# Batch 0's attention by blocks of 128 features in a fused attention and gated MLP kernel

## What is computed

```python
def _attn_ref(q, k, v):                       # [8, 8, 576, 64] each
    q_s = np.exp(q - np.max(q, axis=-1, keepdims=True))
    q_s = q_s / (np.sum(q_s, axis=-1, keepdims=True) + 1e-09)     # softmax over a head's 64 features
    k_s = np.exp(k - np.max(k, axis=2, keepdims=True))
    k_s = k_s / (np.sum(k_s, axis=2, keepdims=True) + 1e-09)      # softmax over the 576 tokens
    kv = np.einsum('bhsd,bhse->bhde', k_s, v)
    return np.einsum('bhsd,bhde->bhse', q_s, kv)
```

## Time and profile before

| | us |
|---|---|
| median of 3 runs | 949.03 (947.65 to 949.77) |
| the profiled execution | 948.56 |
| its span, first to last instruction | 946.8 |
| PE busy in the span | 923.9 (98%) |
| DVE, ACT, POOL busy | 601.5, 374.9, 361.9 |

### The profile page before, as it was taken

One profiled execution on the slowest core, in us unless ns is written; L12 is line 12 of the kernel. 1 busy time (PEld: TensorE's weight loads), 2 busy tenths in 40 slices (PEclk: granted clock), 3 DMA queues, 4 the chain that ended last, 5 costly groups with the idle time before them and its releaser, 6 DMA issues.

```text
span 946.8 us, 14688 instructions
## 1 busy us (share of the span) xinstructions
PE 923.9 (98%) x5980; PEld 864.1 (91%) x5980; DVE 601.5 (64%) x943; ACT 374.9 (40%) x564; POOL 361.9 (38%) x230
## 2 busy tenths in 40 slices
PE   6899899999999999999999998999999999999998
PEld 5799799899999998999999997999998989999987
DVE  6667666657746666576355797866667666667660
ACT  3561433524524335245234254533434333434331
POOL 4985545446426444464204133322222222232320
PEclk8899999999999999999999999999999999999999
DMA  8815425134061151330412302020202020200001
GB/s 256 251 48 178 134 51 193 37 100 158 12 200 56 45 194 41 99 109 12 134 64 82 111 13 73 12 84 23 73 23 73 23 73 23 84 23 22 25 23 55
DMA packets 50482, 77.84 MB, mean 82 GB/s; under 512 B 4336, under 2 KB 22768, under 8 KB 49520
## 3 DMA queue, kind: packets, MB, share of 16 engines
q1 hardware_dynamic: 45808, 67.48, 22.6%
q10 hardware_dynamic: 4608, 9.44, 2.7%
HBM read 56.97 MB, written 18.89 MB: 80 GB/s over the span
## 4 chain that ended last, share of the span: by engine, by line
PE 89%; DVE 6%; DMA 2%; issue 1%; ACT 1%; POOL 1%; SPq 0%; ACTq 0%; DVEq 0%; POOLq 0%
PE psum L452 51%; PE psum L444 29%; PE psum L510 3%; PE psum L593 2%; PE psum L486 2%; PE psum L545 1%; DMA plain_arena<-in_q 1%; DVE plain_arena L1322 1%; DVE split_arena L1304 1%; DMA x_dram<-plain_arena 1%; DVE plain_arena L1133 0%; DVE plain_arena L1246 0%; DVE split_arena L1462 0%; DVE plain_arena L1320 0%; DVE plain_arena L1215 0%
## 5 line engine op out<-in xcount | busy, mean ns | idle before, releaser
L452 PE MATMUL psum<-split_arena 128*128 128x288 f32 x4032 | 559.0, 297 | 6.0 <-DVE split_arena L1201 2.9
L452 PEld LDWEIGHTS psum<-split_arena 128*128 128x128 f32 x4032 | 545.9, 189 | 12.6 <-DVE split_arena L1201 3.2
L444 PE MATMUL psum<-split_arena 128*128 128x512 f32 x1248 | 298.3, 393 | 2.7 <-DVE split_arena L1462 2.6
L444 PEld LDWEIGHTS psum<-split_arena 128*128 128x128 f32 x1248 | 232.2, 189 | 49.8 <-DVE split_arena L1462 3.5
L1614 POOL TENSOR_TENSOR plain_arena<-plain_arena 128x576 f32<-128x576 f32 x64 | 107.4, 1678 | 281.6 <-ACT plain_arena L915 281.6
L1325 DVE SCALAR_TENSOR_TENSOR plain_arena<-plain_arena 128x576 f32<-128x576 f32 x64 | 96.2, 1503 | 2.2
L1320 DVE TENSOR_SCALAR plain_arena<-plain_arena 128x576 f32<-128x576 f32 x64 | 36.0, 563 | 90.1 <-ACT plain_arena L909 90.1
L1555 POOL TENSOR_TENSOR plain_arena<-plain_arena 128x576 f32<-128x576 f32 x32 | 46.5, 1453 | 110.6 <-DVE plain_arena L1259 110.6
L909 ACT ACTIVATE plain_arena<-psum 128x576 f32<-128x576 f32 x64 | 41.6, 650 | 105.4 <-PE psum L452 74.4
L915 ACT ACTIVATE plain_arena<-plain_arena 128x576 f32<-128x576 f32 x64 | 43.7, 683 | 43.5 <-DVE split_arena L1462 40.4
L1462 DVE TENSOR_TENSOR split_arena<-plain_arena,split_arena 128x576 fp32r<-128x576 f32 x64 | 53.2, 832 | 10.9 <-ACT split_arena L921 10.0
(11 more groups left out here) (80 smaller groups left out, 787.0 us busy)
## 6 DMA issues: line engine op xcount, KB each, us to landing
x_dram<-plain_arena ACTq DMA_DIRECT2D x32, 288.0 KB, 2.1
plain_arena<-x_dram SPq DMA_DIRECT2D x8, 1152.0 KB, 5.7
out_rows<-plain_arena SPq DMA_DIRECT2D x36, 256.0 KB, 2.0
plain_arena<-in_v SPq DMA_DIRECT2D x32, 256.0 KB, 3.3
plain_arena<-in_kT SPq DMA_DIRECT2D x7, 1152.0 KB, 8.0
plain_arena<-in_q SPq DMA_DIRECT2D x7, 1024.0 KB, 5.7
plain_arena<-in_k SPq DMA_DIRECT2D x7, 1024.0 KB, 5.6
plain_arena<-in_w_in SPq DMA_DIRECT2D x8, 512.0 KB, 5.8
```

What stands on the lines that cost most here:

```text
L444: mm = e.matmul(out, stat[s], mov[m], start=first and n == 0, stop=last and n == 2, skip_group_check=True)
L452: mm = e.matmul(out[:, h, 0:NH], stat[s], mov[m][:, h * NH:(h + 1) * NH], start=first and n == 0, stop=last and n == 2, skip_group_check=True)
```

## The change

Only batch 0's attention and what is loaded for it are rewritten. Four things are different.

1. Loading. SP issues, for each block d, kT (128 features x 576 tokens), q and v of the block's 128 columns from two new inputs laid out by block (`q_first`, `v_first`, 128 x 5 x 128, the tail's missing rows filled with repeated ones), and the right half of `w_in`'s rows. The left halves follow. `w_in` is split into its two halves for `hi_w` and `lo_w` too.
2. k. DVE takes the maximum along the free axis of kT, ACT exponentiates with the negated maximum as bias, PE turns the exponentiated block once, and ACT (four tiles) and DVE (the tail) copy it out of PSUM.
3. Per block, the value product (5 matmuls into one bank), the inverse of the sums, the halves of kv (with the scale applied in the same instructions), q's chain and its turning, the piece of x, and with it `v_part(0, 0, [d])` follow each other. `v_part(0, 1)` comes at the end in one piece, since all pieces of x use its banks.
4. Batch 1. `load_kT(1)` moves behind `load_q(1)` and `W_SG[1]`, because kT of batch 0 now lies in its place; the load of `W_SG[0]` no longer waits.

Loading, cut:

```diff
-            for u in range(NU):
-                j, n, rows = UNITS[u][0], len(UNITS[u]), rows_of(u)
-                e.dma_start(kn[0:rows, j:j + n, :],
...
-            for j in range(NJ):
-                load_v(0, j)
             for d in range(DT):
-                load_w(W_IN[d], w_in_raw[d])
+                e.dma_start(k_view[:, d, :], kT[0, d * P:(d + 1) * P, :]).then_inc(kT_first_in[d], 16)
+                e.dma_start(qs_first[:, d, :, :], q_first[d].rearrange("p (j c) -> p j c", j=NJ)).then_inc(q_first_in[d], 16)
+                e.dma_start(vs_first[:, :, d, 0:P], v_first[d].rearrange("p (j c) -> p j c", j=NJ)).then_inc(v_first_in[d], 16)
+                load_w(W_IN[0][d], w_in_raw[0][d])
+            for d in range(DT):
+                load_w(W_IN[1][d], w_in_raw[1][d])
             load_w(W_SG[2], w_sg_raw[2])
-            e.wait_ge(kv_step, NJ - 1)
             load_w(W_SG[0], w_sg_raw[0])
-            load_kT(1)
             load_q(1)
             e.wait_ge(w_lo, 2)
             load_w(W_SG[1], w_sg_raw[1])
+            load_kT(1)
             load_k(1)
```

```diff
+            def turn_first_k(d):
+                e.wait_ge(k0_exp, d + 1)
+                if d > 0:
+                    e.wait_ge(k0_main, d)
+                for j in range(NJ - 1):
+                    mm = e.transpose(ek_turned[:, j * P:(j + 1) * P], k_view[:, d, j * P:(j + 1) * P], ident)
+                mm.then_inc(k0_turned, 1)
+            def turn_first_q(d):
+                e.wait_ge(q0_norm, d + 1)
+                if d > 0:
+                    e.wait_ge(q0_lo, d)
...
+            def kv_first_block(d):
...
+                for j in range(NJ):
+                    mm = e.matmul(kv_first, kn[:, j, d * P:(d + 1) * P], vs_first[:, j, d, :],
+                                  start=j == 0, stop=j == NJ - 1, skip_group_check=True)
+            def x_first(d):
+                e.wait_ge(kv0_lo, 2 * d + 2)
+                e.wait_ge(q0_lo, d + 1)
+                if d > 0:
+                    e.wait_ge(x_lo, d)
...
+            def exp_first_k(d):
+                e.wait_ge(k_neg, d + 1)
+                e.activation(k_view[:, d, :], k_view[:, d, :], ACT.Exp, bias=kmax[:, d:d + 1]).then_inc(k0_exp, 1)
...
-                raw = qsum_first if b == 0 else qsum
...
+                e.tensor_scalar(qsum[:, cols], qsum[:, cols], EPS_SOFTMAX, None, ALU.add).then_inc(q0_chain, 1)
...
```

508 lines of the change are left out of this document (307 added, 201 removed).

## The result

The changed kernel takes 952.6 us (median of 20 runs, 949.3 to 958.3), the kernel before 948.0 (20 runs, 946.0 to 951.7): ratio 1.0049, 95% interval 1.0036 to 1.0061. **It is slower by 4.6 us**, within the range, but not the 949.5 of the forecast: it went the way of the slower rival. The profiled execution took 952.57, its span is 950.6 us (execution 948.56 and span 946.8 before).

The account below looks back on a forecast made before the run. PE bounds the kernel (busy 923.9 of 946.8 us); the 6.7 us gained at u is waited away, the mixing starting 0.6 later. 948.56 + 0.6 = 949.2, median plus 0.6 is 949.6; forecast 949.5, range 944.5 to 954.0.

Parts of the forecast that it names:

- slower rival: First attention: q's last turning at 31.2, PE at 1.2 GHz, kT costs 4.6; 954.3 us, decides from 29.2; chance 0.30.
- queue: Batch 1's transfers: kT(1) behind q adds 2.8 us in full, so the maxima's read-back lands at 51.2.
- From sub_k on: POOL, ACT, PE to first mixing: sub_k(1, 0) at 51.4, lo_vn at 54.8, last four matmuls at 65.1, 0.6 us later.
- PE waits away what u gains: Between u and first mixing: u starts 6.7 us earlier at 40.8, but PE idles 6.4 us, from 53.7 to 60.1.
- the length of the stage: Batch 0's first attention: x pieces from 15.7 to 29.6, last turning of q from 27.3 to 27.9.
- the 30 that I had named as a sign of being wrong: Batch 1's q load: expected near 28; before 25 or behind 30 would show the prediction wrong.
- I take DMA as no limit of this stage: First attention's loads: fourth block there by 22, its parts used from 16 to 25, so transfers don't limit.
- PE's pace: First attention: last turning of q at 27.3 to 27.9; PE at half clock all along, the upper bound, gives 31.2.
- The stage is quicker: First attention: q's last turning at 24.5, everything from load_q(1) 3.4 earlier, mixing's tail at 61.7; 945.8 us, chance 0.20.
- The maxima aren't last: Batch 1's transfers overlap so sub_k is not waited for and u's 6.7 us stay: 942.3 us, chance 0.07.
- The addition of the epsilon: DVE, batch 0's q sums, read from SBUF not PSUM: 0 to 1.26 us per block; counted 0, up to 1.3 in range.
- The read-back's landing: Batch 1's maxima back from DRAM: 4.5 us by the trace row, against 2.6 by the skill page.

Follow-up runs that it names:

- experiment 1: Changed kernel with batch 1's kT issued ahead of its q, once batch 0's last k tail is turned: 950.95 us, 1.0033 to the kernel before.
- Experiment 8: Changed kernel with block d's left half of w_in loaded behind kT and q of block d+1: 948.92 us, 1.0020 to the kernel before.
- after: The changed kernel as it is, in its profiled execution (952.57 us, span 950.6): median 952.6 us, 1.0049 to the kernel before.
- experiment 2: Changed kernel with POOL's first subtraction of batch 1, sub_k(1, 0), behind the three lo_vn: 951.46 us, 1.0042 to the kernel before.
- experiment 3: Changed kernel with PE turning k's last tail and making its value product ahead of v_part(0, 0, [0]): 952.33 us, 1.0050 to the kernel before.
- experiment 6: Changed kernel with kT(1) ahead of q(1) and sub_k(1, 0) behind the three lo_vn: 950.76 us, 1.0031 to the kernel before.
- Experiment 7: Changed kernel, first attention's last third reordered: v_part(0, 0, [0]) behind x_first(2), turn_first_q(3) ahead; POOL's scale_first_q(2) ahead of lo_w(0, 1): 949.89 us, 1.0022 to the kernel before.
- experiment 5: Changed kernel with 24 one-column matmuls ahead of PE's first turning: 954.4 us, 1.0080 to the kernel before.
- experiment 9: Changed kernel with q's sums for blocks 0 to 2 written to PSUM and read there for the epsilon: 950.80 us, 1.0041 to the kernel before.
- experiment 11: Changed kernel with kT(1) ahead of q(1), the first attention's last third reordered, and w_in's left halves loaded later: 947.76 us, 1.0004 to the kernel before.
- Experiment 10: Changed kernel with 14 matmuls of 128x128 ahead of PE's first turning: 951.37 us, 1.0042 to the kernel before.
- experiment 12: Kernel of experiment 11 with 14 identity matmuls (4 of one column, 10 of 128) ahead of PE's first turning: 947.81 us, 0.9993 to the kernel before.

## Why the prediction was right or wrong

**What held.** The *queue*: kT's price was to be 2.8; q to read-back grew from 15.9 to 18.4 (2.5), and experiment 1 gives 2.5 back. *From sub_k on*: `lo_vn` 3.2 behind `sub_k`'s start (3.4 forecast), the second normalised v another 3.2 on, the tail 10.3 behind `lo_vn` (10.25), 24 matmuls in 4.96 (4.85). The mixing's wait ends on POOL's and ACT's chain, and the granted clock is 0.57 from 62 to 66, near the level of 1.2 GHz. *PE waits away what u gains*: it stood 0.65 and 3.08 us, 3.7 where 6.4 was forecast, since u began at 45.10 and not at 40.8. The first value product was at 6.98 (6.7 forecast).

**The step that failed is the first: the length of the stage.** The pieces of x start at 17.83, 24.32, 30.22 and 33.51; I had 15.7, 22.2, 26.4 and 29.6. The last turning of q is at 31.10 and not 27.3, above the 29.2 from which I let the slower case decide, and `load_q(1)` was issued at 31.83, behind the 30 that I had named as a sign of being wrong. That the time lies in the range, which is 9.5 us wide, owes something to luck: part of what makes it up (below) is in no term of the sum. Two terms of the stage were wrong.

- *"I take DMA as no limit of this stage".* I looked at the fourth block, where it holds, and not at the second, whose kT stands behind a block's q, v and half of w_in. DVE waited 1.9 for it and started at 8.75. Experiment 8 takes half of w_in from its way, and the first x is 1.75 earlier.
- *PE's pace.* I priced it as fast, with half clock all along as the far bound. It had two paces in one stage, as the rows at 10.37 and 20.10 show. The change from one to the other falls on the trace's records of the clock: in after the first one begins at 18.02 us and grants 1.00, and PE is slow up to there and fast behind it. In experiments 1, 2, 3, 6 and 7 the first record begins at 17.1 to 17.3, and PE is slow in the value product of 13 to 16; in 5, 8, 9 and 11 it begins at 10.3 to 11.5, and PE is fast there. With PE fast from there on, in the changed kernel's order (5, 8, 9, 10), the last turning starts at 27.6 to 28.3: **the forecast's 27.3 is the case in which PE is fast from the second block on, and the changed kernel as profiled is not in it.** Experiment 10 shows the pace by itself: load_q(1) 2.8 earlier.

What decides how early PE gets fast is not shown. It goes with the arrival of kT: over the kernels with nothing put ahead of PE's first turning, DVE's second maximum of k started at 8.22 to 8.77 where PE is still slow in the value product (after, 1, 2, 3, 6, 7) and at 6.9 to 7.9 where it is fast there (8, 9, 11). But experiment 5 lies at 8.12, experiment 10 at 8.24, and both are fast, and experiment 12, with kT early (7.22) and matmuls ahead, is slow again at 11.84.

The hand-over that I had not seen comes on top: POOL does a low half of w_in ahead of `scale_first_q(2)`, PE stands 1.9 us, the clock falls to 0.61, and `v_part` takes 2.76 ahead of k's tail. Experiment 7 shortens the wait to 1.09, moves `v_part`, and the time is 2.6 us less. The wait alone does not bring the clock down: experiment 8 has it too, at full clock, and its `v_part` takes 1.52.

```profile
22.04 0.76 PE L478 MATMUL psum<-plain_arena 128*128 128x128 f32 x5 [1.91 <-POOL plain_arena L1663]
22.00:26.00 4.00, 3.54 (x22) 2.99 (x23) 2.32 (x6) 2.31 (x4) 3.22 (x3) 1.00 0.00 0
```

**From there by the forecast's own terms.** q(1) 3.9 later, the read-back 0.3 less for the queue and 1.2 less for its landing (3.3, forecast 4.5): `sub_k` 2.3 behind forecast, at 53.66, and the mixing 2.1, at 67.16. 0.6 forecast plus 2.1 is the 2.7 measured there.

**What the sum did not have** is all that comes behind. I let everything follow the mixing one for one. It does not. This is by how many us PE is behind the kernel before (minus: ahead of it) at the same work, in the profiled executions; the times are those of the kernel before:

| | mixing's last four, 64.47 | second piece of x of batch 1, 106.62 | the same of batch 2, 169.83 | in the second MLP, 582.32 | span |
|---|---|---|---|---|---|
| after | 2.7 | 2.0 | 3.4 | 3.9 | 3.8 |
| experiment 1 | 2.8 | 0.4 | 2.3 | 2.3 | 2.3 |
| experiment 8 | -0.3 | -3.1 | -1.4 | 0.0 | 0.0 |
| experiment 11 | -0.9 | -3.7 | -1.7 | -0.2 | -0.2 |
| experiment 12 | -1.3 | -1.7 | -1.7 | -1.6 | -1.6 |

Between the first two columns PE waits for what hangs on batch 2's q and on a store of x1, and returns at either level of the clock. The kernel before returns at 0.63 (from 103.4 to 106.7), after at 0.50, and experiments 1, 8 and 11 at 1.00: the 12 matmuls of `v_part` take 4.50, 3.72 and 2.9 us. The last wait is shorter too (2.92 before, 2.04 to 1.61 in the three). Together these three win 2.4 to 2.9 there. Between the next two a store meets an instruction packet. It costs after 1.4 us and experiments 1, 8 and 11 1.6 to 1.9, and experiment 12, whose packet was moved, nothing. The change puts other instructions into PE's stream, and so other places for the packets; this is a part of the 4.6 us that has nothing to do with attention. The last loss, 1.5 of what experiments 8 and 11 had won, is mostly the clock once more, near 575: PE waits 1.97 us in the kernel before and 1.98 in experiment 8, and goes on at different levels (first row before, second row experiment 8).

```profile
573.40:578.00 4.60, 3.34 (x19) 2.85 (x19) 4.60 (x6) 3.15 (x6) 1.76 (x1) 1.00 0.00 0
573.40:578.00 4.60, 4.58 (x19) 4.26 (x20) 4.60 (x6) 1.95 (x3) 1.76 (x1) 0.64 0.00 0
```

**The rivals.** "Slower" had the right place, the last turning of q at 31.2, and one right half, PE at 1.2 GHz with its pauses; its kT at 4.6 was wrong, and the end at 954.3 was close since the packet filled the hole. Its chance of 0.30 was too small against 0.43. "The stage is quicker" is what experiments 8 and 11 made of it. They were 3.1 and 3.7 ahead of the kernel before at 107 and end at 948.9 and 947.8, not at 945.8, since the packet's store and the clock near 575 take it back. "The maxima aren't last" is what experiment 6 reaches, with 950.8 in place of 942.3: behind the maxima stand the deviation of v and u itself, so 6.7 us were never there to be had.

**The addition of the epsilon.** It took 0.17, 0.60, 0.29 and 0.51 in the four blocks, 0.9 more than out of PSUM, inside the 0 to 1.3 that I gave; 0.44 of it is on DVE's path. The Trainium skill, page "SBUF — State Buffer", section "SBUF: two separate sides", has a GpSimd operation and a DVE operation in a two-port mode, or with two inputs in SBUF, block each other on a shared port pair. The trace agrees, and experiment 9 shows that reading from PSUM is enough to escape (0.17 beside POOL), although the result goes to SBUF.

**The read-back's landing.** It came 3.3 us (after), 4.5 (before) and 5.0 (experiment 1) behind the issue. The Trainium skill, page "DMA: Bandwidth & Descriptors", section "Anatomy of one DMA — SWDGE (gpsimd) path", would give 2.6; that section is about transfers that GpSimd issues, and this one is issued by SP. None of the three agrees.

**What stays open.** How often PE is slow up to 18 us in the changed kernel: each kernel has one trace, and only the spread speaks (949.3 to 958.3 for it, 950.6 to 952.3 with 14 matmuls ahead). Why, after waits of one length, the clock falls in one kernel and stays up in another (at 25, 103 and 575). Why the read-back's landing varies from 3.0 (experiment 2) to 5.0.

## What to carry to other kernels

When a stage is rebuilt, price its first hand-overs against the order of its transfers and not against their sum: here moving loads of 256 KB behind what is needed next gave back 2.7 of the 4.6 us. A stage in which PE waits often has no single price per matmul: give it both levels of the clock, and let the range follow. A gain at one place is not a gain at the end: follow PE through the later batches, where one wait and the level of the clock behind it moved PE by up to 2.9 us. And an engine's instruction count is itself a change: before explaining a new gap far behind the edit, look whether an instruction packet met the transfer there.

## What the runs showed that I had not expected

**A granted clock of 1.00 can stand for a stretch without a record.** In after four turnings took 1.11 at 10.37 and 0.66 at 20.10, while the row of the clock says 1.00 for both. The trace's first record of the clock begins at 18.02; for the time before it there is none, and the row then prints 1.00. The slow pace is that of the lower level: ten rows of the value product took 2.50 at 14.05 in after and 2.50 at 11.84 in experiment 12, where the clock is on record at 0.50. That PE stood at 1.2 GHz up to the first record is inferred from these equal times. The rows of the kernel before up to 13.5 us have to be read in the same way: its first record begins at 10.29. 14 matmuls of 128x128 from 1.61 to 6.8, themselves slow (0.37 each), put the turnings behind them to 0.60 to 0.66. 24 matmuls of one column, done in 1.34 us, left the first turnings at 1.12.

```profile
8.00:12.00 4.00, 2.63 (x11) 1.92 (x10) 3.10 (x9) 1.72 (x4) 1.23 (x2) 1.00 1.07 368
24.00:28.00 4.00, 4.00 (x17) 3.30 (x16) 1.19 (x3) 2.40 (x4) 3.13 (x3) 0.61 0.00 0
```

(After: stretch, its length, busy time of PE, PEld, DVE, ACT and POOL with their counts, granted clock, share of DMA, GB/s.)

**PE's instructions come by DMA, in packets that other transfers feel.** The page of after lists `q8 instruction: 47, 0.77, 0.4%`, 47 packets of 16 KB for 11944 matmuls and weight loads, one for about 254 of them. A store of 288 KB beside which one starts landed 3.7 us behind its issue (after) to 4.4 (experiment 2); in before the next addition could write its place 2.3 behind the issue. 96 instructions more moved the one at 165.0 to 158.5, 56 more moved it to 161.0 (experiment 10), and in experiment 12 the one of experiment 11 from 160.0 to 156.5. After's packet at 165.0 has its row in experiment 5. What is taken from one store's way can be put into another's.

**Small operations of DVE in SBUF wait for POOL.** In after three of v's moments, which take 0.14 to 0.16 elsewhere, took 1.94, 1.07 and 1.65 and ended at 48.8, 49.8 and 56.3, each within 0.1 of the end of one of POOL's subtractions; the moments of the first unit took from 45.36 to 50.36, those of the next from 50.87 to 53.08.
